# A recurrence with two expert mixtures on one core: how the first groups of the preparation are inverted and negated

## The chip, the cores and the metric

The kernel runs on one core of a Trainium2 chip. The metric is the device time of one execution in microseconds. The time before is the median of 3 runs, 847.18 us (846.09 to 848.04).

## The reference

```python
def _attn_ref(q, k, v, a_re, a_im):          # all (4, 8, 768, 48): B, H, S, D
    mag = np.sqrt(a_re * a_re + a_im * a_im)
    scale = np.minimum(mag, 0.999) / (mag + 1e-06)
    a_re_n, a_im_n = (a_re * scale, a_im * scale)
    for t in range(S):                        # S_re, S_im: (B, H, D, D), zero at first
        ar, ai = (a_re_n[:, :, t, :, None], a_im_n[:, :, t, :, None])
        new_re = ar * S_re - ai * S_im
        new_im = ar * S_im + ai * S_re
        kv = np.einsum('bhd,bhe->bhde', k[:, :, t], v[:, :, t])
        S_re, S_im = (new_re + kv, new_im)
        y[:, :, t] = np.einsum('bhd,bhde->bhe', q[:, :, t], S_re)
...
x = attn_out.transpose(0, 2, 1, 3).reshape(B * S, H * D)     # 3072 x 384
x = _moe_ref(x, ...)     # 8 experts, top 1 by x @ w_gate, relu(x @ w1) @ w2, skipped where x @ w_skip <= 0
return _moe2_ref(x, ...) # 8 experts, top 1 by xn @ en.T / tau, both normed: en = emb / (norm(emb) + 1e-6)
```

## The kernel before, in words

The recurrence is not run step by step on the 48x48 states. Time is cut into 24 units of 128 steps. A first block, the **preparation** (`running_products`), computes for every unit and head the running product of the normed complex numbers a from the unit's start. A second block, attention, uses these products to turn queries and keys, and two blocks of expert mixtures follow. The change is all inside the preparation; the four blocks run one after the other, with a barrier between the preparation and attention.

The preparation has 128 lanes in its partitions, with 72 segments in each (PSEG), and walks over the 128 steps of a unit for all segments at once. The steps are cut into 12 groups of 4, 8, nine times 12, and 8 steps (`sizes`). A ring of four slots holds groups; each step has three planes in it, imaginary, real and negated imaginary (IM, RE, NEG). For group g:

1. SP loads the imaginary and real planes (`load`); for g >= 4 it first waits until group g - 4 has been copied out (`spread`).
2. ScalarE squares both planes (`squares`). Their sum is made by VectorE for groups 0 to 2 (`add_squares`; EARLY is 3) and by TensorE from group 3 on: a batch of 12 matmuls with the identity (8 for the last group).
3. ScalarE takes the root (`roots`), which gives the magnitude. The inverse is made as exp(-ln(mag + eps)), two ScalarE operations (`inverses`). The root and Ln/Exp are in two table sets, so ScalarE changes its table twice per group.
4. VectorE improves this inverse by one Newton step (`check`, `improve`), multiplies it with the clipped magnitude (`clip`), and scales both planes of the ring in place (`scale`).
5. ScalarE writes the negated imaginary plane (`negate`).
6. VectorE does the steps of the group (`step(t)`, four operations of 144 and 72 elements: product and sum for two halves of the segments). The first step of a group waits for its negated plane (`negated`).
7. ScalarE copies the finished planes to `A` (`spread_out`).

The order on every engine is written out by hand. VectorE does group g's steps with the four parts of group g + 1 between them. ScalarE does in iteration g: squares(g+2), spread_out(g-1), roots(g+2), inverses(g+2), negate(g+1). Ahead of the loop ScalarE does squares(0), squares(1), roots(0), roots(1), the embedding's square sum and root, inverses(0), inverses(1), negate(0). VectorE does add_squares(0), add_squares(1), the five small operations of `embed` (L757 to L765, lanes 0 to 7 only), and the four parts of group 0. TensorE turns the embedding behind the batch of group 3 and waits for `embed` there. GpSimd sets constants and at last (L598) fills 32 lanes of the part of `A` beyond the first 72 segments with ones; SP waits for that (`gap_set`) at the block's end.

In the profile: L606 squares, L615 and L618 roots, L623 and L625 Ln and Exp, L629 negate, L636 spread_out, L686 TensorE's batches, L707 check, L712 improve, L717 clip, L724 scale, L742 and L746 the two halves of a step, L752 add_squares, L765 the last operation of `embed`.

Of the kernel before, what the change touches and what calls it, by code (L numbers as in the profile page):

```python
# [464 lines left out]
def running_products(nc, A, a_end, qk, turner, load_qk, load_v, a, w_route, emb, tau, ident, causal, after,  # L465
# [14 lines left out]
    EARLY = 3  # L480
# [3 lines left out]
    with ExitStack() as ctx:  # L484
# [46 lines left out]
        def flat(t, g):  # L531
            return t[:, g % 2, 0:sizes[g] * PSEG]
# [33 lines left out]
        @block.gpsimd  # L566
        def _(pool):
            pool.memset(eps[:, :], 1e-6)
            pool.memset(tiny[:, :], 1e-34).then_inc(eps_set, 1)
            pool.memset(ident[:, :], 0.0).then_inc(consts, 1)  # L570
            pool.wait_ge(consts, 1)
            pool.affine_select(out=ident[:, :], in_=ident[:, :], compare_op=ALU.not_equal, fill=1.0,
                               base=0, pattern=[[-1, P]], channel_multiplier=1).then_inc(consts, 1)
            pool.memset(turner[:, :, :], 0.0).then_inc(wr_clear, 1)
            pool.memset(qk[:, :, :, :], 0.0).then_inc(qk_clear, 1)
            pool.memset(causal[:, :], 1.0)
            pool.memset(after[:, :], -1.0)
            pool.memset(resets[:, :], 1.0)
            pool.memset(ones[:, :], 1.0).then_inc(consts, 1)
            pool.iota(iota[:, :], [[1, P]], base=0, channel_multiplier=0, allow_small_or_imprecise_dtypes=True)  # L580
            pool.iota(iota_b[:, :], [[1, P]], base=0, channel_multiplier=0, allow_small_or_imprecise_dtypes=True)
            pool.iota(part_no[:, :], [[0, 1]], base=0, channel_multiplier=1, allow_small_or_imprecise_dtypes=True)
            pool.iota(token_hi[:, :], [[P, UNITS]], base=-PAD, channel_multiplier=0,
                      allow_small_or_imprecise_dtypes=True)
            pool.iota(down[:, :], [[-1, E]], base=E, channel_multiplier=0, allow_small_or_imprecise_dtypes=True)
            pool.wait_ge(consts, 3)
            pool.affine_select(out=causal[:, :], in_=causal[:, :], compare_op=ALU.is_ge, fill=0.0,
                               base=0, pattern=[[1, P]], channel_multiplier=-1)
            pool.affine_select(out=after[:, :], in_=after[:, :], compare_op=ALU.is_ge, fill=0.0,
                               base=0, pattern=[[-1, P]], channel_multiplier=1)  # L590
            pool.memset(resets[:, :].rearrange("p (e u) -> p e u", u=UNITS)[:, :, 0], 0.0)
            pool.wait_ge(wr_clear, 1)
            for hh in range(2):
                rows = slice(LANE1 * hh, LANE1 * hh + D)
                pool.tensor_copy(turner[rows, :, D * hh:D * (hh + 1)],
                                 ident[rows, rows].unsqueeze(1).to_broadcast([D, G, D])).then_inc(consts, 1)
                pool.wait_ge(consts, 4 + hh)
            pool.memset(A[LANE1 // 2:LANE1, :, PSEG:SEG, :], 1.0).then_inc(gap_set, 1)  # L598

        @block.scalar  # L600
        def _(act):
            def squares(g):
                act.wait_ge(a_loaded[g % RING], 16 * (g // RING + 1))
                if g > 1:
                    act.wait_ge(summed, g)
                act.activation(square_of(g), ring[:, g % RING, 0:sizes[g], IM:RE + 1, :], ACT.Square  # L606
                               ).then_inc(squared, 1)
# [13 lines left out]
            def inverses(g):  # L621
                act.wait_ge(rooted, g + 1)
                act.activation(flat(recip, g), flat(mag, g), ACT.Ln, bias=eps[:, :]).then_inc(logged, 1)  # L623
                act.wait_ge(logged, g + 1)
                act.activation(flat(recip, g), flat(recip, g), ACT.Exp, scale=-1.0).then_inc(exped, 1)  # L625

            def negate(g):
                act.wait_ge(scaled, g + 1)
                act.activation(ring[:, g % RING, 0:sizes[g], NEG, :], ring[:, g % RING, 0:sizes[g], IM, :],  # L629
                               ACT.Copy, scale=-1.0).then_inc(negated, 1)  # L630
# [19 lines left out]
            act.preload_act_table_set("sqrt_and_others")  # L650
            act.wait_ge(eps_set, 1)
            squares(0)
            squares(1)
            roots(0)
            roots(1)
            act.wait_ge(small_loaded, 32)
            act.activation(embj[:, :], embs[:, :], ACT.Square, accum_out=embn[:, 1:2]).then_inc(emb_step, 1)
            act.wait_ge(emb_step, 2)
            act.activation(embn[:, 2:3], embn[:, 1:2], ACT.Sqrt).then_inc(emb_step, 1)
            act.preload_act_table_set("natural_log_exp_and_others")  # L660
            inverses(0)
            inverses(1)
            negate(0)
            for g in range(GROUPS):
                if g + 2 < GROUPS:
                    squares(g + 2)
                if g > 0:
                    spread_out(g - 1)
                if g + 2 < GROUPS:
                    roots(g + 2)  # L670
                    act.preload_act_table_set("natural_log_exp_and_others")
                    inverses(g + 2)
                if g + 1 < GROUPS:
                    negate(g + 1)
            spread_last()

# [24 lines left out]
        @block.vector  # L701
        def _(dve):
            def check(g):
                dve.wait_ge(exped, g + 1)
                if g > 0:
                    dve.wait_ge(scaled, g)
                dve.scalar_tensor_tensor(factor[:, 0:sizes[g] * PSEG], flat(mag, g), 1e-6, flat(recip, g),  # L707
                                         ALU.add, ALU.mult).then_inc(newton, 1)
# [11 lines left out]
            def scale(g):  # L720
                dve.wait_ge(newton, 3 * g + 3)
                both = ring[:, g % RING, 0:sizes[g], IM:RE + 1, :]
                by = factor[:, 0:sizes[g] * PSEG].rearrange("p (t s) -> p t s", t=sizes[g])
                dve.tensor_tensor(both, both, by.unsqueeze(2).to_broadcast([P, sizes[g], 2, PSEG]), ALU.mult  # L724
                                  ).then_inc(scaled, 1)

            def here(t, plane, planes, c):
                g = group_of[t]
# [23 lines left out]
                dve.tensor_tensor(total[:, 0:sizes[g] * PSEG].rearrange("p (t s) -> p t s", s=PSEG),  # L752
                                  square_of(g)[:, :, 0, :], square_of(g)[:, :, 1, :], ALU.add).then_inc(summed, 1)

            def embed():
                dve.wait_ge(emb_step, 1)
                dve.tensor_scalar(embn[:, 1:2], embn[:, 1:2], 1e-34, None, ALU.max).then_inc(emb_step, 1)  # L757
                dve.wait_ge(emb_step, 3)
                dve.tensor_scalar(embn[:, 3:4], embn[:, 2:3], 1e-6, None, ALU.add).then_inc(emb_step, 1)
                dve.wait_ge(emb_step, 4)  # L760
                dve.tensor_tensor(embn[:, 1:2], embn[:, 3:4], embn[:, 0:1], ALU.mult).then_inc(emb_step, 1)
                dve.wait_ge(emb_step, 5)
                dve.reciprocal(embn[:, 2:3], embn[:, 1:2]).then_inc(emb_step, 1)
                dve.wait_ge(emb_step, 6)
                dve.tensor_scalar(embj[:, :], embs[:, :], embn[:, 2:3], None, ALU.mult).then_inc(emb_step, 1)  # L765

            add_squares(0)
            add_squares(1)
            embed()
            for part in (check, improve, clip, scale):  # L770
                part(0)
            for g in range(GROUPS):
                parts = [check, improve, clip, scale] if g + 1 < GROUPS else []
                for n in range(1 if g == 0 else 0, sizes[g]):
                    step(starts[g] + n)
                    if parts and n >= 1 and (sizes[g] < SPAN or n % 2 == 1):
                        parts.pop(0)(g + 1)
                    if g + 2 < EARLY and n == 2:
                        add_squares(g + 2)
                for part in parts:  # L780
                    part(g + 1)
                if g == 5:
                    dve.wait_ge(emb_T, 1)
                    dve.tensor_copy(wr2[:, :, :], bank[7][:, 0:KC * E].rearrange("p (c e) -> p c e", c=KC))
                    dve.wait_ge(wr_clear, 1)
                    for hh in range(2):
                        rows = slice(LANE1 * hh, LANE1 * hh + D)
                        dve.tensor_copy(turner[rows, :, 2 * D + E + 1:],
                                        bank[5 + hh][rows, 0:G * E].rearrange("p (g e) -> p g e", g=G))

                if g == 1:
                    dve.memset(a_end[0:ROWS], 0.0).then_inc(ended, 1)
# [900 lines left out]
```

## Time and profile before

| | us |
|---|---|
| median of 3 runs | 847.18 |
| profiled execution | 848.65 |
| its span | 846.6 |
| VectorE, first step (step(1)) | 15.29 |
| first step of group 1 (step(4)) | 25.41 |
| first step of group 2 (step(12)) | 38.18 |
| first step of group 3 (step(24)) | 51.70 |
| attention's first ScalarE activation | 166.21 |

The span is from the first to the last instruction of one execution. The profile lists, for each engine, when an instruction starts, its length, and how long the engine was idle before it and for whom it waited. TensorE was busy for 678.4 us of the span, VectorE for 656.4, ScalarE for 496.0 and GpSimd for 271.7. These are averages over stages with different limits: in the preparation TensorE does little.

### The profile page before, as it was taken

What the parts mean: (1) busy time and instruction counts of PE and PEld (TensorE: products, weight loads), DVE (VectorE), ACT (ScalarE), POOL (GpSimd) and SP (SyncE); (2) the same over time, 40 slices, a digit from 0 to 9 for tenths busy, and PEclk for the clock granted to TensorE, in tenths of its full rate; (3) what the DMA queues carried; (4) which work ended last, traced back from release to release, by engine and by line L of the source; (5) the groups of instructions that cost most, each with busy time, mean ns of one, the idle gap of its engine ahead of it and who ended that gap; (6) DMA issues with size and microseconds to landing.
All of it is one profiled execution on the core that took longest, in us unless ns stands there. A gap on an engine that the chain in (4) does not pass through costs nothing.

```text
span 846.6 us, 18780 instructions
## 1 busy us (share of the span) xinstructions
PE 678.4 (80%) x7172; PEld 637.7 (75%) x7172; DVE 656.4 (78%) x1285; ACT 496.0 (59%) x710; POOL 271.7 (32%) x234
## 2 busy tenths in 40 slices
PE   0334251079989989955999999999999999999996
PEld 0223131068877878844999999999999999999996
DVE  5799999969999999976767757756788577567661
ACT  5888888556566565543556455555655455545541
POOL 5000000011111111104778655442243226875412
PEclk9865665559999999985999999999999999999999
DMA  7121210018742333238575665756755665655720
GB/s 182 42 84 43 85 54 16 0 36 152 156 113 85 103 100 94 84 47 268 184 231 192 201 235 180 257 155 235 245 187 199 213 212 184 235 188 182 278 91 28
DMA packets 80219, 123.96 MB, mean 146 GB/s; under 512 B 14826, under 2 KB 62454, under 8 KB 79968
## 3 DMA queue, kind: packets, MB, share of 16 engines
q1 hardware_dynamic: 71392, 106.48, 41.3%
q0 software_dynamic: 8768, 16.72, 5.8%
q8 instruction: 34, 0.56, 0.3%
q14 instruction: 25, 0.20, 0.1%
HBM read 111.35 MB, written 13.84 MB: 148 GB/s over the span
## 4 chain that ended last, share of the span: by engine, by line
PE 48%; DMA 2%; issue 2%; POOL 1%; DVE 1%; ACT 0%; POOLq 0%; SPq 0%; DVEq 0%
PE banks L1252 22%; PE banks L1269 21%; DMA raw<-w2a 2%; PE banks L1227 2%; PE banks L1234 2%; PE banks L1237 1%; POOL over_table L1157 1%; PE banks L1218 1%; DMA out<-mix_y,lists 1%; ACT w_hi L850 0%; SPq L833 0%; DVE w_lo L855 0%; POOLq L1177 0%; POOL out L1148 0%; DVE mix_hT_lo L1545 0%
## 5 line engine op out<-in xcount | busy, mean ns | idle before, releaser
L1252 PE MATMUL banks<-mix_xT_hi,w_hi 128*128 128x240 f32 x576 | 163.4, 284 | 2.9 <-DVE mix_xT_lo L1554 2.9
L1269 PE MATMUL banks<-mix_hT_hi,w_hi 128*128 128x240 f32 x576 | 163.2, 283 | 0.5 <-DVE mix_hT_lo L1545 0.4
L1252 PE MATMUL banks<-mix_xT_lo,w_hi 128*128 128x240 f32 x576 | 159.7, 277 | 0.0
L1252 PE MATMUL banks<-mix_xT_hi,w_lo 128*128 128x240 f32 x576 | 159.2, 276 | 0.0
L1269 PE MATMUL banks<-mix_hT_lo,w_hi 128*128 128x240 f32 x576 | 158.6, 275 | 0.0
L1269 PE MATMUL banks<-mix_hT_hi,w_lo 128*128 128x240 f32 x576 | 158.1, 274 | 0.0
L686 PE MATMUL banks<-sq,ident 128*128 128x288 f32 x104 | 47.2, 633 | 90.2 <-ACT sq L606 90.2
L1252 PEld LDWEIGHTS banks<-mix_xT_hi,w_hi 128*128 128x128 f32 x576 | 110.1, 191 | 3.2 <-issue 3.2
L1252 PEld LDWEIGHTS banks<-mix_xT_lo,w_hi 128*128 128x128 f32 x576 | 110.3, 191 | 0.0
L686 PEld LDWEIGHTS banks<-sq,ident 128*128 128x128 f32 x104 | 31.2, 311 | 104.9 <-ACT sq L606 66.4
L1252 PEld LDWEIGHTS banks<-mix_xT_hi,w_lo 128*128 128x128 f32 x576 | 110.2, 191 | 0.0
L1269 PEld LDWEIGHTS banks<-mix_hT_hi,w_hi 128*128 128x128 f32 x576 | 109.1, 189 | 1.0 <-DVE mix_hT_lo L1545 0.9
L1269 PEld LDWEIGHTS banks<-mix_hT_lo,w_hi 128*128 128x128 f32 x576 | 109.2, 190 | 0.0
L1269 PEld LDWEIGHTS banks<-mix_hT_hi,w_lo 128*128 128x128 f32 x576 | 109.1, 189 | 0.0
L1314 ACT ACTIVATE mix_hT_hi<-banks 128x480 fp32r<-128x480 f32 x96 | 54.8, 571 | 90.5 <-PE banks L1252 90.3
L1545 DVE SCALAR_TENSOR_TENSOR mix_hT_lo<-banks,mix_hT_hi 128x480 fp32r<-128x480 f32 x96 | 62.8, 654 | 55.2 <-ACT mix_hT_hi L1314 55.1
L855 DVE TENSOR_TENSOR w_lo<-raw,w_hi 128x1536 fp32r<-128x1536 f32 x48 | 83.9, 1750 | 1.5 <-ACT w_hi L845 1.5
L861 DVE TENSOR_TENSOR w_lo<-raw,w_hi 128x1536 fp32r<-128x1536 f32 x48 | 82.1, 1750 | 0.0
L845 ACT CAST w_hi<-raw 128x1536 fp32r<-128x1536 f32 x48 | 70.5, 1472 | 14.9 <-DMA raw<-w1a 10.6
L1157 POOL DMA_INDIRECT over_table<-mix_record,mix_position x48 | 68.6, 1429 | 26.5 <-issue 26.5
L207 POOL TENSOR_TENSOR qk<-sqs 112x512 f32 x22 | 28.1, 1279 | 152.4 <-DVE rk L306 152.4
L1554 DVE TENSOR_TENSOR mix_xT_lo<-banks,mix_xT_hi 128x384 fp32r<-128x384 f32 (+1 forms) x48 | 25.2, 531 | 66.1 <-ACT mix_xT_hi L1321 65.9
(216 smaller groups left out, 1513.6 us busy)
## 6 DMA issues: line engine op xcount, KB each, us to landing
raw<-w1b SPq DMA_DIRECT2D x16, 1536.0 KB, 7.7
raw<-w2b SPq DMA_DIRECT2D x16, 1536.0 KB, 7.2
raw<-w1a SPq DMA_DIRECT2D x8, 1536.0 KB, 7.6
raw<-w2a SPq DMA_DIRECT2D x8, 1536.0 KB
ring<-a SPq DMA_DIRECT2D x9, 864.0 KB, 4.8
qk<-q SPq DMA_DIRECT2D x48, 96.0 KB, 2.3
qk<-k SPq DMA_DIRECT2D x48, 96.0 KB, 2.3
vt<-v SPq DMA_DIRECT2D x24, 192.0 KB, 2.5
```

The costliest lines, as they stand in the source:

```text
L207: pool.tensor_tensor(qk[0:ROWS, bass.ds(u & 1, 1), 2].rearrange("p o n -> p (o n)"), sqs[0:ROWS, 0], sqs[0:ROWS, 1], ALU.add).then_inc(nor ...
L686: last = pe.matmul(banks[:, c, 0:STEP * PSEG].rearrange("p (t s) -> p t s", t=STEP), ident[:, :], sq[:, c * STEP:(c + 1) * STEP, j, :], st ...
L845: act.copy(self.part(self.hi1[:, slot.b], half), self.part(self.raw1[:, :, :], half)).then_inc(slot.ph.hi1_ready, 1)
L855: dve.tensor_tensor(self.part(self.lo1[:, slot.b], half), self.part(self.raw1[:, :, :], half), self.part(self.hi1[:, slot.b], half).bitcas ...
L861: dve.tensor_tensor(self.part(self.lo2[:, slot.b], half), self.part(self.raw2[:, :, :], half), self.part(self.hi2[:, slot.b], half).bitcas ...
L1157: pool.indirect_dma_start(ph.table.rearrange("p (c e) -> (p c) e", e=2), bass.IndirectOffsetOnAxis(ap=position[:, u:u + 1], axis=0), recor ...
L1227: last = pe.transpose(turns[s][:, c * P:(c + 1) * P], rows[:, slot.b, s, c * P:(c + 1) * P], ident[:, :])
L1252: last = pe.matmul(pU[g % TURNS][:, n * N:(n + 1) * N], w1p[m][:, b, c, f * P:(f + 1) * P], xT[s][:, c, 0:N], start=(c == 0 and (s, m) == ...
L1269: last = pe.matmul(turned(c)[:, 0:N], w2p[m][:, b, f, c * P:(c + 1) * P], hT[s][:, f, 0:N], start=(f == 0 and c % 2 == 0 and (s, m) == PAS ...
L1314: act.activation(hT[0][:, 2 * g:2 * g + 2, 0:N], pU[g % TURNS][:, 0:2 * N].rearrange("p (c t) -> p c t", c=2), ACT.Relu).then_inc(ph.h_hi, 1)
L1545: dve.scalar_tensor_tensor(hT[1][:, 2 * g:2 * g + 2, 0:N], pU[g % TURNS][:, 0:2 * N].rearrange("p (c t) -> p c t", c=2), 0.0, hT[0][:, 2 * ...
L1554: dve.tensor_tensor(xT[1][:, :, cols], turns[s][:, 0:DM].rearrange("p (c t) -> p c t", c=KC)[:, :, 0:m], xT[0][:, :, cols].bitcast(F32), A ...
```

## The change

Group 0 gets its inverse from VectorE's reciprocal, in place of ScalarE's Ln and Exp and VectorE's Newton step. The negated planes of groups 0, 1 and 2 are written by VectorE (as -2x + x) and no longer by ScalarE. The embedding's operations stand later in the queues of VectorE and ScalarE. ScalarE's preparation order is rearranged, one table load is issued ahead of the wait that it stood behind, and the parts of groups 1 and 2 stand at other places between VectorE's steps. GpSimd's clearing of lanes waits for the first step of group 2.

```diff
@@ gpsimd
+            pool.wait_ge(added[0], starts[2])
             pool.memset(A[LANE1 // 2:LANE1, :, PSEG:SEG, :], 1.0).then_inc(gap_set, 1)
@@ scalar
             def inverses(g):
                 act.wait_ge(rooted, g + 1)
                 act.activation(flat(recip, g), flat(mag, g), ACT.Ln, bias=eps[:, :]).then_inc(logged, 1)
-                act.wait_ge(logged, g + 1)
+                act.wait_ge(logged, g)
...
             squares(0)
+            roots(0)
             squares(1)
-            roots(0)
-            roots(1)
             act.wait_ge(small_loaded, 32)
             act.activation(embj[:, :], embs[:, :], ACT.Square, accum_out=embn[:, 1:2]).then_inc(emb_step, 1)
-            act.wait_ge(emb_step, 2)
-            act.activation(embn[:, 2:3], embn[:, 1:2], ACT.Sqrt).then_inc(emb_step, 1)
+            roots(1)
             act.preload_act_table_set("natural_log_exp_and_others")
-            inverses(0)
             inverses(1)
-            negate(0)
             for g in range(GROUPS):
                 if g + 2 < GROUPS:
                     squares(g + 2)
                 if g > 0:
                     spread_out(g - 1)
+                if g == 0:
+                    act.preload_act_table_set("sqrt_and_others")
+                    act.wait_ge(emb_step, 2)
+                    act.activation(embn[:, 2:3], embn[:, 1:2], ACT.Sqrt).then_inc(emb_step, 1)
                 if g + 2 < GROUPS:
                     roots(g + 2)
                     act.preload_act_table_set("natural_log_exp_and_others")
                     inverses(g + 2)
-                if g + 1 < GROUPS:
+                if EARLY <= g + 1 < GROUPS:
                     negate(g + 1)
@@ vector
             def check(g):
-                dve.wait_ge(exped, g + 1)
+                dve.wait_ge(exped, g)
...
+            def invert_first():
+                dve.wait_ge(rooted, 1)
+                dve.tensor_scalar(flat(recip, 0), flat(mag, 0), 1e-6, None, ALU.add).then_inc(newton, 1)
+                dve.wait_ge(newton, 1)
+                dve.reciprocal(factor[:, 0:sizes[0] * PSEG], flat(recip, 0)).then_inc(newton, 1)
+
+            def negate(g):
+                dve.wait_ge(scaled, g + 1)
+                plane = ring[:, g % RING, 0:sizes[g], IM, :]
+                dve.scalar_tensor_tensor(ring[:, g % RING, 0:sizes[g], NEG, :], plane, -2.0, plane, ALU.mult, ALU.add
+                                         ).then_inc(negated, 1)
...
-            def embed():
+            def bound_embed():
                 dve.wait_ge(emb_step, 1)
                 dve.tensor_scalar(embn[:, 1:2], embn[:, 1:2], 1e-34, None, ALU.max).then_inc(emb_step, 1)
+
+            def embed():
                 dve.wait_ge(emb_step, 3)
...
             add_squares(0)
+            invert_first()
             add_squares(1)
-            embed()
-            for part in (check, improve, clip, scale):
-                part(0)
+            clip(0)
+            scale(0)
+            negate(0)
             for g in range(GROUPS):
                 parts = [check, improve, clip, scale] if g + 1 < GROUPS else []
+                if 0 < g + 1 < EARLY:
+                    parts.append(negate)
                 for n in range(1 if g == 0 else 0, sizes[g]):
                     step(starts[g] + n)
-                    if parts and n >= 1 and (sizes[g] < SPAN or n % 2 == 1):
+                    if parts and (n >= 3 if g == 1 else n % 2 == 1 and g > 1):
                         parts.pop(0)(g + 1)
-                    if g + 2 < EARLY and n == 2:
-                        add_squares(g + 2)
+                if g == 0:
+                    bound_embed()
                 for part in parts:
+                    if g == 0 and part is scale:
+                        add_squares(2)
                     part(g + 1)
+                if g == 1:
+                    embed()
```

## Rows read from the trace of the kernel before

**Rows 1.** Waits of VectorE, 38 to 165 us: us in total, times, longest.
```profile
DVE prod L742 <- ACT ring L629: 1.7, 1, 1.7
```

**Rows 2.** Busy time by stretch: batches 3, 4 to 10, 11; group 2; batch 4.
```profile
core 0: us, PE busy (x) PEld busy (x) DVE busy (x) ACT busy (x) POOL busy (x), PEclk, DMA share, GB/s
27.05:31.69 4.64, 4.63 (x13) 3.19 (x14) 4.64 (x14) 1.04 (x2) 0.00 (x0) 1.00 0.54 154
32.50:130.00 97.50, 38.35 (x84) 25.57 (x84) 95.75 (x365) 84.78 (x67) 0.00 (x0) 0.65 0.21 61
133.80:138.10 4.30, 4.21 (x8) 2.52 (x8) 4.30 (x17) 4.04 (x3) 0.00 (x0) 0.50 0.00 0
38.18:51.70 13.52, 5.14 (x12) 3.44 (x12) 13.52 (x52) 11.13 (x10) 0.00 (x0) 0.63 0.23 65
39.70:45.00 5.30, 5.14 (x12) 3.44 (x12) 5.30 (x20) 2.98 (x3) 0.00 (x0) 0.62 0.21 57
```

**Rows 3.** Order of time on VectorE: start, length, instruction, [idle before <- releaser].
```profile
4.68 0.46 DVE L752 TENSOR_TENSOR total<-sq_early 128x288 f32<-128x288 f32 x1 [4.68 <-ACT sq_early L606]
7.56 0.76 DVE L752 TENSOR_TENSOR total<-sq 128x576 f32<-128x576 f32 x1 [2.42 <-ACT mag L615]
...
10.62 2.02 DVE L765 TENSOR_SCALAR embj<-embs,embn 8x384 f32<-8x384 f32 x1
...
15.29 0.53 DVE L742 TENSOR_TENSOR prod<-ring 128x144 f32<-128x144 f32 x2 [0.51 <-ACT ring L629]
...
16.02 0.75 DVE L707 SCALAR_TENSOR_TENSOR factor<-mag,recip 128x576 f32<-128x576 f32 x1
...
18.08 1.05 DVE L752 TENSOR_TENSOR total<-sq 128x864 f32<-128x864 f32 x1
...
20.56 1.36 DVE L724 TENSOR_TENSOR ring<-ring,factor 128x1152 f32<-128x1152 f32 x1
25.41 0.53 DVE L742 TENSOR_TENSOR prod<-ring 128x144 f32<-128x144 f32 x2 [3.49 <-ACT ring L629]
...
26.14 0.52 DVE L742 TENSOR_TENSOR prod<-ring 128x144 f32<-128x144 f32 x2
...
38.18 0.53 DVE L742 TENSOR_TENSOR prod<-ring 128x144 f32<-128x144 f32 x2 [1.70 <-ACT ring L629]
...
51.70 0.53 DVE L742 TENSOR_TENSOR prod<-ring 128x144 f32<-128x144 f32 x2
...
133.31 0.53 DVE L742 TENSOR_TENSOR prod<-ring 128x144 f32<-128x144 f32 x2
```

**Rows 4.** Order of time on ScalarE, columns as in rows 3.
```profile
6.93 0.52 ACT L615 ACTIVATE mag<-total,tiny 128x288 f32<-128x288 f32 x1
...
12.27 0.76 ACT L623 ACTIVATE recip<-mag,eps 128x576 f32<-128x576 f32 x1
13.06 0.68 ACT L625 ACTIVATE recip<-recip 128x576 f32<-128x576 f32 x1
...
19.21 1.28 ACT L615 ACT_TABLE_LOAD   x1 [2.42 <-DVE total L752]
...
24.71 0.67 ACT L629 ACTIVATE ring<-ring 128x576 f32<-128x576 f32 x1
25.28 1.63 ACT L606 ACTIVATE sq<-ring 128x1728 f32<-128x1728 f32 x1
...
38.05 1.63 ACT L606 ACTIVATE sq<-ring 128x1728 f32<-128x1728 f32 x1
...
50.42 0.91 ACT L629 ACTIVATE ring<-ring 128x864 f32<-128x864 f32 x1
...
131.86 0.91 ACT L629 ACTIVATE ring<-ring 128x864 f32<-128x864 f32 x1
```

**Rows 5.** Groups by line on VectorE: count | busy us, mean ns | idle before.
```profile
L1479 DVE RECIPROCAL mix_weight<-mix_weight 128x24 f32<-128x24 f32 x3 | 0.9, 303 | 0.1
L1478 DVE TENSOR_SCALAR mix_weight<-mix_weight 128x24 f32<-128x24 f32 x3 | 0.5, 178 | 0.1
L763 DVE RECIPROCAL embn<-embn 8x1 f32<-8x1 f32 x1 | 0.2, 151 | 0.0
```

**Rows 6.** DMA issues, 0 to 60 us: count, KB each, median us to landing.
```profile
ring<-a SPq DMA_DIRECT2D x5, 864.0 KB, 5.7
```

**Rows 7.** Order of time on GpSimd, columns as in rows 3.
```profile
7.22 5.21 POOL L598 MEMSET A<- 32x6144 f32 x1
```

## The prediction

> **What bounds the kernel now.** I read the page's engine table first, then the waits, the stretches by group and the order of instructions on VectorE and ScalarE for the first 60 us. All edits lie in the preparation, which ends at 166 us of an 846.6 us span; behind it comes code that the change leaves alone and that starts when the preparation ends. So the question is by how much the preparation's end moves.
>
> Two regimes are to be seen. From group 2's first step (38.18) on VectorE has no gap: its wait list for 38 to 165 us holds one entry, the 1.7 us that end there [rows 1], and a group of twelve steps takes 13.52 us, all of it busy [rows 2]. Before 38 us the chain is a zigzag between VectorE and ScalarE: step(1) starts only at 15.29, step(4) at 25.41, step(12) at 38.18, the last two after waits of 3.49 and 1.70 us for ScalarE's negated plane [rows 3].
>
> Beside the saturated VectorE a second loop runs with almost the same period: ScalarE squares a group, TensorE sums it, ScalarE takes the root, inverts and negates. ScalarE waits in it for nothing but the matmul batch. Negate(3) ends at 50.42 + 0.91 = 51.33 [rows 4]; step(24), which needs it, starts at 51.70 [rows 3]. The slack is 0.37 us, so a saving of VectorE alone meets ScalarE at once. In the six groups after it the same reading gives slacks between 0.49 and 0.87; the last is 133.31 - (131.86 + 0.91) = 0.54 [rows 3, 4].
>
> **The change, part by part.**
>
> *Up to step(1).* Add(0) still ends at 4.68 + 0.46 = 5.14 [rows 3]. Now roots(0) comes before squares(1) on ScalarE: it takes 0.52 [rows 4] and ends at 5.69 with 0.03 of handing over, before the data of group 1 lets squares(1) begin at 5.86, so the swap costs nothing. VectorE goes on at 5.72 with the added 1e-6, a TENSOR_SCALAR of 288 elements. One of 24 elements took 178 ns [rows 5], a two-input one of 288 took 0.46 [rows 3], and one beside GpSimd's long memset took 2.02 [rows 3]; GpSimd then has only ops of some 0.2 us, so I take 0.40 and keep 2.0 as the far end. End 6.12.
>
> The reciprocal of 288 elements is the unknown term. Rows: one element 151 ns, 24 elements 303 ns, and a plain op on the same 24 elements 178 ns [rows 5]. The line through the first two has 6.6 ns per element and gives 0.303 + 264 x 0.0066 = 2.05. With the excess over the plain op, 125/24 = 5.2 ns, plus the plain 1.0 ns, it is 1.95. I take 2.0. Bounds: 0.46 if it ran like any other op, and 3.6 if all 303 ns belonged to the elements (288 x 12.6). It ends at 6.15 + 2.0 = 8.15.
>
> The Trainium skill speaks for a slower one: VectorE: DVE Perf Modes, section "First, the fixed hardware budget", has the reciprocal as a divide step repeated eight times; as an estimate, eight cycles at its 0.96 GHz make 2.4 us for 288, and the time would be 0.4 us above mine. The rows are nearer 6 cycles.
>
> Behind it stand add(1) 0.76, clip(0) 0.46, scale(0) on 576 elements 0.76 and the new negate(0) 0.46, with 0.03 between dependent ones and 0.05 of overlap where none depends: step(1) starts at 10.6 instead of 15.29. Add(1) stands now behind the reciprocal, 1.1 us later than its squares, which end at 7.02, would allow. Gone are the embedding's five small ops, of which the last took 2.02 [rows 3], check(0) and improve(0), and ScalarE's Ln and Exp for group 0.
>
> *Up to step(4).* Three steps of 0.73 [rows 3] and bound_embed's 0.15 bring VectorE to 13.0. ScalarE: roots(1) from 8.9 to 9.7, table load 1.28, Ln 0.76 and Exp 0.68 [rows 4] end at 12.45, so check(1) finds its input with 0.5 to spare. Check, improve, clip (0.75 each), add(2) 1.05, scale(1) 1.36 and negate(1) 0.75 [rows 3], which now stand in one row, end at 18.4: step(4) at 18.4 instead of 25.41. Squares(2) ends at 14.0, ahead of add(2) at 15.3.
>
> *Up to step(12).* From 25.41 to 38.18 VectorE's own work was 12.77 - 1.70 = 11.07. It gains negate(2) (1.0) and embed (about 1.0: five small ops, the last without the memset beside it). VectorE would be at step(12) at 18.4 + 11.07 + 2.0 = 31.5, instead of 38.18.
>
> *ScalarE's loop*, which decides from there. Add(2) starts at 18.08 now, at 15.25 then: 2.83 earlier. The table load of 1.28 that came after its end (19.21) is issued before it: 1.28. ScalarE has no negate(1) (25.28 - 24.71 = 0.57, its 0.67 less 0.10 of overlap) and no negate(2) (by the same overlap 0.91 - 0.10 = 0.81) [rows 4]. So squares(4) starts 5.5 us before its 38.05, at 32.5, and negate(3), still ScalarE's, ends at 51.33 - 5.5 = 45.8. VectorE's own work would have let step(24) start at 31.5 + 13.5 = 45.0: it waits 0.8 us here. Step(24) starts at 45.8 instead of 51.70, 5.9 us earlier.
>
> *From step(24) on* the period is VectorE's again. The slacks shrink by 5.9 - 5.5, some 0.35 us, to between 0.15 and 0.5, all above zero, so nothing more is lost and nothing gained. Group 4's load is released by the first spread-out, which stands right behind squares(3) on ScalarE and so moves to about 23.4; its squares come at 32.5, so it keeps 9 us for a transfer whose median is 5.7 [rows 6].
>
> *The clearing of lanes on GpSimd.* The 5.21 us memset [rows 7] moves from 7.22 to behind step(12), to about 32. SP waits for it only at the end of the block, 120 us later, and nothing else stands behind it in GpSimd's queue. What it costs VectorE's steps beside it: the row is add(1), two inputs of 576 elements, which ran at 7.56 within the memset and took 0.76, no more than its size asks. I take nothing, with 5.2 us as the far end.
>
> Here a page speaks against the change. The Trainium skill, GPSIMD Engine Reference, section "Specifications", says that GpSimd contends with VectorE instructions with two SBUF inputs, which all steps are; by that rule VectorE would stand still for the memset (rival A). The trace disagrees with its 0.76 us; SBUF: State Buffer, section "Who interferes with whom", limits it to a GpSimd instruction that reads.
>
> *Sum:* 2.83 + 1.28 + 0.57 + 0.81 + 0.37 (slack used up) = 5.9. The profiled execution took 848.65 with its span of 846.6; it would be 842.8. The median of the runs is 847.18, so 841.3.
>
> *Bounds of the sum.* The reciprocal passes on one to one, since add(2) hangs on it: at 0.46 the gain would be 7.0 (squares(1) then holds add(1) back), at 3.6 it is 4.3, and a held-up TENSOR_SCALAR also makes it 4.3. TensorE's clock: batch 3 ran at granted 1.00 in 4.64 us, batch 4 at a mean of 0.62 in 5.14 [rows 2]; 1.00 is 2.4 GHz and 0.50 is 1.2. Batch 4 comes at 34.2 now, and only 2.4 us behind the embedding's transposes; at the upper level it would save 0.5, and the gain is 6.4.
>
> **Rivals.**
>
> A: the memset stops the steps. Place: group 2, 32 to 37 us. VectorE loses 5.2 us, of which 0.8 is slack; gain 5.9 - 4.4 = 1.5, time 845.7. Against it stands the 0.76 of add(1); for it, the 2.02 us of the embedding's last op, whose end at 12.64 lies just behind the memset's at 12.43. But that is a one-input op.
>
> B, the slower side: TensorE's batches lengthen. The last batch, 8 matmuls at granted 0.50, took 4.21, so twelve at 1.2 GHz take 6.3. Batches 3 to 10 took 4.63 + 38.35 = 43.0 [rows 2]. Were all eight at the lower level, ScalarE's loop would lose 50.5 - 43.0 = 7.5 us, of which the slack left at the last of them, 0.2, absorbs little: 5.9 - 7.3 = -1.4, time 848.6. It decides against the change from a mean of 0.76 us per batch on. The idle time before a batch stays about 8 us, which speaks against it, as does 1.00 for batch 3.
>
> C: the saving isn't passed on, because a part of ScalarE's early chain that I price at the queue's order (the embedding's data for the Square at 7.0, where the row shows only that it was there at 9.04; check(3) with 0.3 us of slack) comes late. The data at 9.0 would make Exp(1) end at 13.3 and cost 0.3 to 1.5 with the waits behind it: gain 4.4, time 842.8.
>
> D: the reciprocal is as cheap as other ops: gain 7.0, time 840.2. Against it: 303 against 178 ns at 24 elements.
>
> E: the edit removes waits that something outside sets, so nothing moves: 847.2. Against it: no wait behind 6 us in the preparation is for a transfer.
>
> **How the numbers follow.** My forecast has 0.68, C 0.10, D 0.07, A 0.08, B 0.03, E 0.04. Range: the likeliest with 4.3 to 6.9 us of gain, that is 840.3 to 842.9, and 0.5 for the spread of the median; upward it reaches to part of the way to A: 839.9 to 843.8. About 0.2% (1.7 us) is what a measurement tells from no change. My forecast, C and D are faster; A at 1.5 us lies at that bound and is split; E is the same; B at 1.4 us slower is split between same and slower. Faster 0.90, same 0.07, slower 0.03.
>
> **What would show it right or wrong.** RECIPROCAL of 128x288 near 2.0 us; step(1) at 10.6, step(4) at 18.4, step(12) at 31.5, a wait of VectorE for negate(3) of 0.8 us ahead of step(24) at 45.8, and none behind it; TENSOR_TENSORs of group 2 at 305 and 230 ns beside the memset (rival A: one of them near 5 us); batches of 5 to 5.6 us (B: 6.3); embed's last op under 0.6 us. The forecast is wrong if VectorE waits again in groups 4 to 9, or if the code behind the preparation takes other than its 846.6 - 165.7 = 681 us.

## The result and the profile after

The changed kernel took 842.51 us (median of 7 runs, 840.67 to 846.96), the kernel before 847.18 in the same comparison: ratio 0.995, 95% interval 0.9934 to 0.9965. The forecast was 841.3 in a range of 839.9 to 843.8. The median fell by 4.7 us where 5.9 stood in the forecast.

VectorE in order of time (start, length, instruction, [idle before <- releaser]); the rows answer to [rows 3]:

```profile
4.70 0.46 DVE L765 TENSOR_TENSOR total<-sq_early 128x288 f32<-128x288 f32 x1 [4.70 <-ACT sq_early L607]
5.76 0.34 DVE L730 TENSOR_SCALAR recip<-mag 128x288 f32<-128x288 f32 x1 [0.60 <-ACT mag L616]
6.13 1.96 DVE L732 RECIPROCAL factor<-recip 128x288 f32<-128x288 f32 x1
8.01 0.70 DVE L765 TENSOR_TENSOR total<-sq 128x576 f32<-128x576 f32 x1
...
10.38 0.53 DVE L755 TENSOR_TENSOR prod<-ring 128x144 f32<-128x144 f32 x2
...
14.86 1.05 DVE L765 TENSOR_TENSOR total<-sq 128x864 f32<-128x864 f32 x1
...
18.01 0.53 DVE L755 TENSOR_TENSOR prod<-ring 128x144 f32<-128x144 f32 x2
...
30.09 0.41 DVE L780 TENSOR_SCALAR embj<-embs,embn 8x384 f32<-8x384 f32 x1
...
30.83 0.44 DVE L755 TENSOR_TENSOR prod<-ring 128x144 f32<-128x144 f32 x2
...
32.60 1.06 DVE L708 SCALAR_TENSOR_TENSOR factor<-mag,recip 128x864 f32<-128x864 f32 x1 [0.31 <-ACT recip L626]
...
46.33 0.53 DVE L755 TENSOR_TENSOR prod<-ring 128x144 f32<-128x144 f32 x2 [1.62 <-ACT ring L630]
...
74.02 0.53 DVE L755 TENSOR_TENSOR prod<-ring 128x144 f32<-128x144 f32 x2 [0.42 <-ACT ring L630]
...
161.58 0.38 DVE L287 MEMSET state<- 128x384 f32 x1 [0.65 <-PEq L484]
```

Steps 1, 4 and 12 start at 10.38, 18.01 and 30.83 (before: 15.29, 25.41, 38.18), without a wait ahead of them. Then ScalarE's loop takes over: step(24) waits 1.62 us for the negated plane and starts at 46.33, and step(48) waits 0.42 once more. The last row is attention's first VectorE instruction, which stood at 166.33: 4.75 us are left of the 7.35 that step(12) had gained. Behind the preparation the profiled execution needed 839.8 - 161.58 = 678.2 us, where the one before needed 680.3; over the profiles below, of kernels whose code there is the same, this part was between 676.8 and 686.9, so single times can't be read to a microsecond, and I read the experiments by the marks of the preparation.

ScalarE and TensorE at the place that decides; same columns:

```profile
16.00 1.01 ACT L616 ACTIVATE mag<-total,tiny 128x864 f32<-128x864 f32 x1 [0.64 <-DVE total L765]
...
20.21 1.63 ACT L607 ACTIVATE sq<-ring 128x1728 f32<-128x1728 f32 x1
...
32.47 1.63 ACT L607 ACTIVATE sq<-ring 128x1728 f32<-128x1728 f32 x1
...
45.39 0.91 ACT L630 ACTIVATE ring<-ring 128x864 f32<-128x864 f32 x1
```
```profile
21.98 4.95 PE L687 MATMUL banks<-sq,ident 128*128 128x288 f32 x12 [21.98 <-ACT sq L607]
...
34.15 5.69 PE L687 MATMUL banks<-sq,ident 128*128 128x288 f32 x12 [2.38 <-ACT sq L607]
```

Roots(2), the first row, starts 0.09 us after add(2) has ended (14.86 + 1.05), with no table load between them: before, the load of 1.28 stood there [rows 4]. No run undoes this part of the change by itself; its 1.28 us is read from these rows. Squares(4) starts at 32.47, and 32.5 was forecast. Batches 3 and 4 are longer than before, 4.95 and 5.69 instead of 4.63 and 5.14 [rows 2], and negate(3) ends at 46.30, not 45.8.

### The profile page after: what moved, and what is told of

It is laid out like the page before. It is cut to its first block, busy times and chain, and to the rows that moved or that the text cites. A ratio compares the mean times of both kernels' runs of the same rounds, so it can differ in the third digit from the quotient of the medians.

```text
span 839.8 us, 18779 instructions
## 1 busy us (share of the span) xinstructions
PE 677.8 (81%) x7172; PEld 637.3 (76%) x7172; DVE 658.2 (78%) x1288; ACT 493.5 (59%) x705; POOL 270.6 (32%) x234
## 4 chain that ended last, share of the span: by engine, by line
PE 49%; DMA 2%; issue 2%; POOL 1%; DVE 1%; ACT 0%; POOLq 0%; SPq 0%; DVEq 0%
PE banks L1274 22%; PE banks L1291 21%; DMA raw<-w2a 2%; PE banks L1249 2%; PE banks L1256 2%; PE banks L1259 1%; POOL over_table L1179 1%; PE banks L1240 1%; DMA out<-mix_y,lists 1%; ACT w_hi L872 0%; SPq L855 0%; DVE w_lo L877 0%; POOLq L1199 0%; POOL out L1170 0%; DVE mix_hT_lo L1567 0%
```

## The experiments

Each is an edit of the changed kernel unless it says otherwise. Where parts of the change are undone, the old lines come back at their old place, and of the edit only the main lines are shown. The kernels ran on different chips: the median of the kernel before was 847.5 us beside experiments 1 to 4, 849.0 beside 5 to 8 and 848.0 beside 9 to 12, so times of different groups are compared by their ratios.

**1. The memset early.**
```diff
-            pool.wait_ge(added[0], starts[2])
```


> The changed kernel with one line undone: GpSimd clears the lanes of A at its old place (from about 7.2 us), not behind step(12). Theory (the memset holds up only one-input VectorE ops such as the embedding's last one, and that now runs at 30 us): step(1) stays at 10.4, step(4) at 18.0, step(24) at 46.3, time within 0.2% of the changed kernel's 842.5. Rival (moving the memset is itself a part of the gain, because it slows VectorE's or ScalarE's early work): step(1) later by 1 us or more and the time up by as much.

Measured: 841.47 us, ratio to before 0.9933 (0.9915 to 0.995). Step(1) 10.40, step(4) 18.03, step(24) 46.98. The early marks stay, as the theory had it; the 0.65 us at step(24) are batches 3 and 4 (5.36 and 5.90), see below. By itself the memset's place is worth nothing.

**2. The embedding's work early.**
```diff
             add_squares(1)
+            bound_embed()
+            embed()
             clip(0)
```
On ScalarE the embedding's root goes back ahead of roots(1), as it stood before.

> The changed kernel with the embedding's work at its early place (behind add(1), ahead of clip(0); its root ahead of roots(1)), the memset still late. Theory: without the memset beside it the work costs VectorE about 1.5 us (four ops of 0.13 to 0.15, the last 0.41, and the wait for ScalarE's root), so step(1) at 11.9 and step(24) at 47.8, time 844.0. Rival (the embedding's early place costs the 2 us and more that it took before, whatever is beside it): step(1) at 13 to 14.5.

Measured: 844.03 us, 0.9956 (0.9943 to 0.997). Step(1) 11.64, step(24) 48.83. It costs 1.26 us at step(1), and its last operation took 0.41. Step(24) is 1.0 later than forecast, because the batches took 11.91 together and not 10.64 (sums below).

**3. Both early** (the edits of 1 and 2).

> Both undone: the embedding's work early and the memset early. Theory: its last op, one input, stands still until the memset ends at about 12.5 us, so step(1) is at about 14.5, 2.6 us later than with the embedding alone early, step(24) at 50.4 and the time 846.6: the two moves are worth together what neither costs alone. Rival (each has a price of its own, they add): step(1) at 11.9, as with the embedding alone, time 844.

Measured: 846.65 us, 0.999 (0.9978 to 1.0003). VectorE's row for the embedding's last operation:

```profile
9.79 2.91 DVE L779 TENSOR_SCALAR embj<-embs,embn 8x384 f32<-8x384 f32 x1
```

It stands until the memset is over; step(1) starts at 14.38, 4.0 us late: 1.26 from the place and 2.7 from the memset, which alone cost nothing. The price belongs to the pair, and either move takes away this part of it.

**4. Group 0 by Ln and Exp.**
```diff
-            invert_first()
             add_squares(1)
+            check(0)
+            improve(0)
             clip(0)
```
On ScalarE `inverses(0)` comes back ahead of `inverses(1)`, with the old wait counts.

> The changed kernel with group 0 inverted as before (ScalarE's Ln and Exp behind the table load, VectorE's check and improve), all else of the change kept. Theory: group 0 then waits for add(1), roots(1) and the table load; Exp(0) ends at 10.9, step(1) starts at 13.7 instead of 10.4, and all of VectorE's and ScalarE's chain shifts by 3.3: step(24) at 49.6, time 845.8. Rival (the reciprocal of 1.96 us is no cheaper than what it replaces, since add(2) and ScalarE's loop decide anyway): step(24) and time move by less than 1 us.

Measured: 845.75 us, 0.998 (0.9967 to 0.9994). Step(1) 13.70, step(4) 21.33, step(24) 50.40. The reciprocal is worth 3.3 us to all that follows: the new way doesn't wait for group 1's squares and roots on ScalarE, nor for the table load ahead of Ln. Step(24) is 0.8 later than forecast, again by the batches (11.39).

**5. The planes of groups 1 and 2 negated by ScalarE.**
```diff
-                if EARLY <= g + 1 < GROUPS:
+                if g + 1 < GROUPS:
                     negate(g + 1)
...
-                if 0 < g + 1 < EARLY:
-                    parts.append(negate)
```


> The changed kernel with the negated planes of groups 1 and 2 on ScalarE again, behind inverses(2) and inverses(3); group 0's stays on VectorE. Theory: ScalarE's loop gets its 0.57 and 0.81 back, and each first step waits for ScalarE again: step(4) at 20.9 instead of 18.0, step(12) at 33.9 instead of 30.8, step(24) at 47.7 instead of 46.3, time 843.9. Rival (moving the planes only trades 2.3 us of VectorE's time for ScalarE's and gains nothing by group 3): step(24) at 46.3 or before.

Measured: 845.61 us, 0.9949 (0.9926 to 0.9971).

```profile
20.94 0.53 DVE L755 TENSOR_TENSOR prod<-ring 128x144 f32<-128x144 f32 x2 [3.73 <-ACT ring L630]
33.75 0.53 DVE L755 TENSOR_TENSOR prod<-ring 128x144 f32<-128x144 f32 x2 [0.88 <-ACT ring L630]
```
```profile
46.02 0.91 ACT L630 ACTIVATE ring<-ring 128x864 f32<-128x864 f32 x1
```

Both first steps wait for ScalarE again, at the places forecast (20.9, 33.9). Step(24) starts at 47.27, 0.4 before the forecast and with no wait: this execution's batches were short (4.69, 5.16), so that VectorE's own 13.52 us decided. ScalarE's loop did get its 1.4 us back: negate(3), the last row, ends at 46.93. In the changed kernel it ended at 46.30 with batches of 10.64 together; with this execution's 9.85 that would be 45.5. The preparation ends at 162.12, 0.5 us later than in the changed kernel's first profile, whose batches were longer. The changed kernel's second profile (experiment 10) ends at 163.10, later than this one. So moving these two planes is worth 2.9 us at step(4) and at step(12), and no gain of it is shown at the end of the preparation; the ratio doesn't tell the two kernels apart either.

**6. Add(2) one place earlier.**
```diff
-                    if g == 0 and part is scale:
+                    if g == 0 and part is clip:
                         add_squares(2)
```


> The changed kernel with add_squares(2) ahead of clip(1), one place earlier on VectorE. Theory (ScalarE's loop decides from group 3 and hangs on add(2)): roots(2) starts at 15.4 instead of 16.0 (the table load and the embedding's root end at 15.36), step(4) stays at 18.0, the wait ahead of step(24) shrinks from 1.6 to 1.0 us, step(24) at 45.7, time down by 0.6. Rival (VectorE decides at group 3): step(24) unchanged.

Measured: 842.79 us, 0.9933 (0.9909 to 0.9958). Roots(2) starts at 15.26 and step(4) at 18.00, as the theory had them, but step(24) at 46.98, later and not earlier: batch 3 took 5.92 and batch 4 6.13, 1.4 us more than in the changed kernel's profile. The place of step(24) missed the forecast; the gain is there ahead of the batches, batch 3 starting at 21.22 instead of 21.98, and the longer batches take more than it.

**7. GpSimd reading beside the steps.**
```diff
-            pool.memset(A[LANE1 // 2:LANE1, :, PSEG:SEG, :], 1.0).then_inc(gap_set, 1)
+            pool.memset(A[LANE1 // 2:LANE1, :, PSEG:SEG, :], 1.0).then_inc(consts, 1)
+            for n in range(2):
+                pool.wait_ge(consts, 6 + n)
+                pool.tensor_copy(A[LANE1 // 2:LANE1, 1, PSEG:SEG, :], A[LANE1 // 2:LANE1, 0, PSEG:SEG, :]
+                                 ).then_inc(consts if n == 0 else gap_set, 1)
```


> The changed kernel with GpSimd reading beside VectorE's steps: behind its memset, in group 2, it copies the cleared lanes twice (32 x 3072 elements each, plane 0 to plane 1, all ones), waiting for each. Theory (only a GpSimd instruction that reads holds up VectorE's two-input ops): steps beside the memset run as ever, a step or part beside each copy is longer by about the copy's length (some 2.6 us each if it copies as fast as it clears), 1.6 us of it lost in the wait ahead of step(24): time up by 3 to 4 us or more. Rival (no two-input op is held up by GpSimd): step(24) at 46.3, time 842.5.

Measured: 843.86 us, 0.9949 (0.9928 to 0.997). GpSimd, then VectorE:

```profile
31.61 5.21 POOL L599 MEMSET A<- 32x6144 f32 x1 [24.33 <-DVE ring L763]
36.88 5.67 POOL L602 COPY A<-A 32x3072 f32<-32x3072 f32 x2
```
```profile
34.43 0.52 DVE L759 TENSOR_TENSOR prod<-ring 128x144 f32<-128x144 f32 x2
...
36.85 3.06 DVE L759 TENSOR_TENSOR prod<-ring 128x144 f32<-128x144 f32 x2
39.84 2.94 DVE L763 TENSOR_TENSOR ring<-prod 128x72 f32<-128x72 f32 x2
```

Beside the memset a pair of products takes 0.52 as ever; beside each copy one pair, first of products and then of sums, takes 3 us, 2.5 more than the 0.52 and 0.37 that such pairs take elsewhere. Step(24) starts at 49.93, 3.6 later, and the preparation ends at 164.50, 2.9 later than in the changed kernel's first profile. The forecast of the time, 3 to 4 us more, missed: the median is 1.1 us above experiment 6 on the same chip, and the runs spread from 841.75 to 851.35. By the rows, the GpSimd instruction that reads holds up the two-input operations and the one that only writes doesn't. The Trainium skill has it so in SBUF — State Buffer, section "Who interferes with whom", and the trace agrees. The unrestricted line of the Trainium skill's GPSIMD Engine Reference, section "Specifications", which I had made into rival A, does not hold for this memset.

**8. TensorE kept at work.**
```diff
+            def busy(n):
+                for _ in range(n):
+                    pe.matmul(bank[4][:, 0:P], ident[:, :], ident[:, :], start=True, stop=True)
...
                 last.then_inc(summed, 1)
+                if g + 1 < GROUPS:
+                    busy(16 if g == 3 else 32)
                 if g == 3:
...
                     last.then_inc(emb_T, 1)
+                    busy(12)
```


> The changed kernel with TensorE kept at work between its batches: 32 matmuls of the identity with itself (128 columns, into an unused bank) behind each batch, 16 and 12 around the embedding's transposes. Nothing else reads them. Theory (the 1.1 us that the gain fell short by is batches 3, 4 and 6 running longer at a lower granted clock while VectorE has no slack left): the granted clock of the batches is near 1.00, each takes 4.7 us or less, step(24) is at 45.3, the second wait is gone, time down by 1.6. Rival (the batch lengths aren't the clock's, or VectorE decides): batches of 5.5, step(24) at 46.3; if the extra matmuls run over, batches start late and the time goes up.

Measured: 841.22 us, 0.992 (0.989 to 0.995).

```profile
21.98 4.79 PE L691 MATMUL banks<-sq,ident 128*128 128x288 f32 x12 [21.98 <-ACT sq L607]
26.61 3.73 PE L682 MATMUL banks<-ident 128*128 128x128 f32 x32
...
34.07 3.11 PE L691 MATMUL banks<-sq,ident 128*128 128x288 f32 x12
37.02 7.31 PE L682 MATMUL banks<-ident 128*128 128x128 f32 x64
45.23 3.18 PE L691 MATMUL banks<-sq,ident 128*128 128x288 f32 x12 [0.90 <-ACT sq L607]
```
The stretch of that last batch, columns as in [rows 2]:
```profile
45.23:48.41 3.18, 3.18 (x14) 2.55 (x15) 3.18 (x15) 3.18 (x2) 0.00 (x0) 1.00 0.00 0
```
```profile
32.45 1.06 DVE L715 SCALAR_TENSOR_TENSOR factor<-mag,recip 128x864 f32<-128x864 f32 x1 [0.16 <-ACT recip L626]
...
44.52 0.53 DVE L762 TENSOR_TENSOR prod<-ring 128x144 f32<-128x144 f32 x2
```

The batches fall to 3.1 to 3.2 us, not to 4.7; batch 3, with nothing ahead of it, doesn't. The waits ahead of step(24) and step(48) are gone. Step(24) starts at 44.52 and the preparation ends at 159.12, 2.5 us before the changed kernel's. I had forecast 45.3 and 1.6: I took 4.6 for a batch at full clock. The changed kernel didn't run on this chip; experiments 10 and 11 repeat the comparison on one.

**9. The kernel before, with the same extra matmuls.**

> The kernel before with the same extra matmuls behind TensorE's batches as in the run that kept TensorE at work. Theory: in the kernel before VectorE has no wait behind step(12), so TensorE's batch lengths are free there: batches 4 to 10 shrink to about 3.2 us as they did in the changed kernel, batch 3, with nothing ahead of it, stays at 4.6 to 5.9, and step(12), step(24) and the time stay (within 0.2% of before). Rival (short batches are worth 2.5 us in any version, through the clock that attention or the mixtures start with): the time falls by 2 us or more.

Measured: 848.24 us, 1.0005 (0.9993 to 1.0017). Batches 4, 5, 7 and 9 took 3.18, batch 3 4.71; batches 6, 8 and 10 did not shrink as forecast (6.13, 4.66 and 4.57). Step(12) stands at 38.25, step(24) at 51.78, the end at 166.38 (before: 38.18, 51.70, 166.33). Batch 4 is 2 us shorter than before and nothing moves: the length of the batches was free in the kernel before and is not any more in the changed one.

**10. The changed kernel again.**

> The changed kernel again, for comparison on the same chip: about 0.995 of before. Batch 3 and batch 4 differ from the first profile's 4.95 and 5.69 by some tenths of a us (the one that undid only the memset's place, with its batch 3 starting at the same 22.0, had 5.36 and 5.90), and step(24) differs from 46.33 by the same.

Measured: 843.09 us, 0.9946 (0.9927 to 0.9964). Batches 5.73 and 6.09, step(24) 47.57, end 163.10. That is 1.2 and 1.5 us later than in its first profile, more than the tenths that I expected.

**11. TensorE kept at work, again.**

> The changed kernel with TensorE kept at work, again, against the changed kernel on the same chip. Theory: VectorE decides alone from step(12) on; step(24) at 44.5 and the preparation's end 2.5 us before the changed kernel's, time 2.5 us (0.3%) below it. Rival (the first comparison was noise): within 1 us of it.

Measured: 841.10 us, 0.9916 (0.9896 to 0.9936). Step(24) 44.87, end 159.47. It has the lowest median of all versions. Against the changed kernel on the same chip it is 2.0 us faster by the medians and 3.6 by the preparation's ends. The two intervals of the ratio to before still overlap, but the slowest of its five runs (842.20) is below the fastest of the changed kernel's six (842.42). One of its batches, batch 7, took 5.93 without a wait behind it.

**12. Four edits together** (those of 6 and 8, and these).
```diff
             pe.wait_ge(consts, 2)
+            pe.wait_ge(squared, 3)
+            busy(40)
...
+                    if g == 1:
+                        negate(2)
                     inverses(g + 2)
...
-                if 0 < g + 1 < EARLY:
+                if g + 1 == 1:
                     parts.append(negate)
```


> The changed kernel with four edits: TensorE kept at work as before and also by 40 extra matmuls ahead of batch 3, add_squares(2) ahead of clip(1), and group 2's negated plane back on ScalarE, between roots(3) and Ln of group 3. Theory: with batch 3 at 3.2 us ScalarE is 2.2 us earlier at roots(3), has room for negate(2) from 28.2 on, and VectorE, now the bound, loses the 1.0 us of its own negate(2): step(12) at 29.8 (30.8 with the plane on VectorE), step(24) at 43.4, the end 1.0 to 1.2 us before the kernel with TensorE kept at work alone, time 3.6 us below the changed kernel. Rival (ScalarE is the bound in group 2): VectorE waits for negate(2) or Exp(3) by the 1 us that it saved, no gain over keeping TensorE at work.

Measured: 842.65 us, 0.9942 (0.9923 to 0.9961). Step(24) 45.99 (43.4 forecast), end 160.58, which is 1.1 later than in experiment 11. It is a miss of my own sizing:

```profile
14.01 10.50 PE L684 MATMUL banks<-ident 128*128 128x128 f32 x80 [14.01 <-ACT sq L607]
24.35 3.08 PE L695 MATMUL banks<-sq,ident 128*128 128x288 f32 x12
```

Each call of this matmul makes two records, so the 40 took 10.5 us. (The batches' calls do as well: a batch of twelve steps is 6 calls in the kernel and the 12 records that I have counted as matmuls throughout.) Batch 3, which the squares would have allowed at 21.2, started at 24.35, and step(12) waited 2.08 us for negate(2). Batch 3 itself took 3.08: with work ahead of it, it is short as well. Whether a fitting number would bring the microsecond that I expected wasn't tried.

**One sum for all of them.** Step(24) follows from two readings, the start of add(2) and the lengths of batches 3 and 4, wherever ScalarE's loop decides. Taken from the changed kernel's 46.33, with add(2) at 14.86 and batches of 10.64 together:

```
kernel                  add(2)   batches 3+4    sum     measured
changed, again          14.92    5.73 + 6.09    47.57   47.57
memset early            14.88    5.36 + 5.90    46.97   46.98
embedding early         16.08    5.79 + 6.12    48.82   48.83
both early              18.81    4.57 + 5.50    49.71   49.71
Ln and Exp              18.18    5.44 + 5.95    50.40   50.40
add(2) earlier          14.07    5.92 + 6.13    46.95   46.98
```

In experiments 5, 7, 8, 11 and 12 VectorE decides at step(24), which starts there without a wait.

## Why the prediction was right, point by point

*Up to step(1): right.* Forecast 10.6, measured 10.38. The reciprocal took 1.96 (2.0 forecast), the TENSOR_SCALAR 0.34 (0.40). The estimate of 2.4 from the Trainium skill, VectorE: DVE Perf Modes, section "First, the fixed hardware budget", was too high; the measurement decides. D is out: it had 0.46 us for the reciprocal.

*Up to step(4) and step(12): right.* 18.01 against 18.4 and 30.83 against 31.5. The first has 0.2 from step(1) and 0.2 from operations that overlap more than I gave them; from step(4) to step(12) VectorE's own work was 12.8 us where I had 13.1. The embedding's last operation took 0.41 (under 0.6 forecast), and the second experiment shows that moving it away was worth 1.3 us, the third that with the memset beside it it was 4.0.

*ScalarE's loop decides from there: right.* VectorE waited at step(24), by 1.62 instead of 0.8.

*The sum: mis-sized in two terms, of opposite sign.* I took the batches over from the kernel before. Add(2) came 3.22 us earlier, not 2.83; that is 0.4 more. Batches 3 and 4 took 10.64 in place of 9.77; that is 0.9 less. Together 5.4 at step(24), where 5.9 stood. That squares(4) stood where it was forecast is luck: add(2) came 0.4 us too early for the forecast and batch 3 took 0.3 too long. The one sentence that failed outright is the next: "nothing more is lost". Step(48) waited again, 0.42; in the changed kernel's second profile both step(36) and step(48) did (0.33 and 0.53), with batches of 5.86 and 5.74 where the slack left was 0.15 to 0.5. At the preparation's end 4.75 of the 5.9 were left in the first profile and 3.2 in the second, and the median of the runs moved by 4.7, the ratio by 4.2. A wait in groups 4 to 9 was one of the two signs that the prediction named for its being wrong, and in this clause it was. The other, code behind the preparation that takes other than 681 us, came as well (678.2) but says nothing: 680.3 in the kernel before and 676.8 to 686.9 in the others is its spread from one execution to the next. So rival B named the right place and had its size wrong: batches 3 and 4 of 5.0 to 6.1, not 6.3, and not all eight. That the batches are the cause of what is missing is shown by experiments 8 and 11, which change TensorE alone and give it back, and by 9, where the same edit gives nothing.

*The clock: wrong, and for a reason of reading.* I read "batch 3 ran at granted 1.00 in 4.64". A batch at 2.4 GHz takes 3.18 (granted 1.00 in experiment 8's row). The last batch of the kernel before, granted 0.50 [rows 2], has records with a median of 687 ns; the 3.18 us batch has 406 (the three numbers of a row are the shortest, the median and the longest, in ns). In the changed kernel the row of batch 3 reads 1.00 too, but its first four records have the lower level's length, and most of its last six have the upper's. The rows are those of the last batch before, of the 3.18 us batch and of batch 3:

```profile
21.98:26.93 4.95, 4.95 (x12) 3.33 (x12) 4.95 (x15) 1.01 (x2) 0.00 (x0) 1.00 0.59 171
```
```profile
L686 PE MATMUL banks<-sq,ident x8: 687/687/847, 133.9 to 137.4; 128*128 128x288 f32 x8
L691 PE MATMUL banks<-sq,ident x12: 406/406/510, 45.2 to 48.0; 128*128 128x288 f32 x12
L687 PE MATMUL banks<-sq,ident x12: 406/687/818, 22.0 to 26.5; 128*128 128x288 f32 x12
L687 PE MATMUL banks<-sq,ident x4: 687/687/818, 22.0 to 23.6; 128*128 128x288 f32 x4
L687 PE MATMUL banks<-sq,ident x6: 406/406/687, 25.0 to 26.5; 128*128 128x288 f32 x6
```

So the batch starts at the lower level and rises within, and in this stretch the granted clock of the row is not to be trusted. That is read from the lengths alone.

My bound "batch 4 at the upper level saves 0.5" had therefore the wrong price too (2 us), and didn't come about: batch 4 took 5.69.

*The memset: right.* Pairs of products beside it kept their 0.52 us, and moving it alone did nothing. A is out. C is out in its main part: the embedding's Square ran at 6.94 with its data there. Its other half, check(3), came true by 0.31 us, and cost nothing where step(24) waited anyway. E is out, since the marks moved as forecast.

*Left open.* The same batch 3 takes 4.69 to 5.92 us in executions that start it at 21.2 to 22.6. What differs is when its records come closer. They start 0.48 us apart at first, in the changed kernel's first profile up to 25.47 and then about 0.25 apart, in the second (5.73 us) up to 26.97, with only one more behind. Why that point moves is not shown.

## What to carry to other kernels

When two loops have nearly the same period, a saving at the start goes to the faster one only until it meets the other: add up the second loop's chain as well, and ask which of its parts the old slack had hidden, since their spread becomes yours. A cost that needs two things beside each other, here VectorE's one-input operation on 8x384 elements beside GpSimd's fill, goes away with either and can't be credited to both. Where a short burst on TensorE stands in such a chain after an idle stretch, look at the durations of its single matmuls as well as at the mean clock of the stretch.

## What the runs showed of the hardware that I had not expected

- A batch of twelve records took 3.1 to 3.2 us in most cases with TensorE at work ahead of it, and 4.6 to 6.1 without. Still, in three of the four profiles with extra matmuls one such batch took 5.9 to 6.1 (and in one of them two others 4.6 and 4.7), so work ahead of it is no guarantee. Batch 3 apart, the granted clock goes with the length: 1.00 for 3.18 us, 0.67 for 4.66, 0.53 for 5.93, 0.50 for 6.13.
- GpSimd's copy stops a two-input VectorE operation for most of its 2.8 us (a pair took 3.06 and 2.94 against 0.52 and 0.37). GpSimd's memset stops none of them, but held up the one-input TENSOR_SCALAR on 8x384 elements until it ended (2.91 us against 0.41). It did not hold up the embedding's operations on one element per lane, which took 0.13 to 0.15 beside it.
- The reciprocal of 288 elements took 1.955 us and that of 24 elements 0.303, which is 6.3 ns for each further element.
